# Transposing keys and queries 128 columns at a time, with an earlier place for them in the attention steps

## The reference

```python
block, window = (32, 16)
k_sum = k.reshape(B, H, nb, block, D).max(axis=3)      # 24 blocks of 32 keys
v_sum = v.reshape(B, H, nb, block, D).mean(axis=3)
scores_l = scale * q @ k.T, kept where |i - j| < window
scores_s = scale * q @ k_sum.T + log(block)
a = softmax over both; out = a @ concat(v, v_sum)
```

## Time and profile before

| engine | busy us | share of the span | instructions |
|---|---|---|---|
| PE (matmul) | 550.4 | 89% | 3031 |
| PEld (weight load) | 453.7 | 74% | 3032 |
| DVE | 299.4 | 49% | 726 |
| ACT | 260.9 | 42% | 509 |
| POOL | 106.3 | 17% | 152 |

### The profile page before, as it was taken

The page is one execution under the profiler, slowest core; times in us unless marked ns, Lnnn a source line. Parts: engine busy times, 40 slices in busy tenths (PEclk is TensorE's granted clock), DMA queues, the critical chain, the costliest instruction groups (busy, mean ns, idle before and its releaser), DMA issues.

```text
span 616.8 us, 10082 instructions
## 1 busy us (share of the span) xinstructions
PE 550.4 (89%) x3031; PEld 453.7 (74%) x3032; DVE 299.4 (49%) x726; ACT 260.9 (42%) x509; POOL 106.3 (17%) x152
## 2 busy tenths in 40 slices
PE   2687878796299999999997999999999999999996
PEld 1576667675178888888885888888888888888884
DVE  3645644554675521255126576674355445344441
ACT  2636656544346412144214455543433333433332
POOL 3253562100711200013101522300000000000000
PEclk9969998985599999999999999999999999999999
DMA  8949695202765541134411633300100000100001
GB/s 175 210 90 202 144 290 143 86 2 69 251 219 191 169 175 34 51 115 162 149 53 53 206 102 103 104 18 18 68 0 0 0 0 0 68 0 0 0 0 68
DMA packets 47790, 58.37 MB, mean 95 GB/s; under 512 B 21448, under 2 KB 33736, under 8 KB 47376
## 3 DMA queue, kind: packets, MB, share of 16 engines
q1 hardware_dynamic: 36464, 24.12, 16.7%
q0 software_dynamic: 8640, 29.53, 14.5%
q10 hardware_dynamic: 2656, 4.34, 2.1%
HBM read 41.83 MB, written 14.94 MB: 92 GB/s over the span
## 4 chain that ended last, share of the span: by engine, by line
PE 84%; ACT 5%; DVE 4%; DMA 3%; issue 2%; SPq 0%; POOL 0%; ACTq 0%; DVEq 0%
PE bank L569 76%; ACT SM L1262 2%; PE bank L573 2%; PE bank L634 2%; PE bank L730 2%; DMA TAU<-in_moe_tau 1%; PE bank L708 1%; DMA x_grouped<-XALL,POS 1%; ACT QT L1225 1%; DVE SM L892 1%; DVE VSUM L877 1%; PE bank L799 1%; DMA XG<-x_grouped 1%; ACT XT L1249 1%; ACT KTC L1219 0%
## 5 line engine op out<-in xcount | busy, mean ns | idle before, releaser
L569 PE MATMUL bank<-X2H,WIH 128*128 (+1 forms) x192 | 77.1, 402 | 2.8 <-DVEq L1184 2.8
L569 PE MATMUL bank<-X2H,WIL 128*128 (+1 forms) x192 | 76.6, 399 | 0.0
L569 PE MATMUL bank<-X2L,WIH 128*128 (+1 forms) x192 | 76.5, 398 | 0.0
L569 PE MATMUL bank<-WOH,GH 128*128 128x512 f32 x192 | 75.7, 394 | 0.0
L569 PE MATMUL bank<-WOL,GH 128*128 128x512 f32 x192 | 75.6, 394 | 0.0
L569 PE MATMUL bank<-WOH,GL 128*128 128x512 f32 x192 | 75.6, 394 | 0.0
L573 PE MATMUL bank<-IDENT,KQRAW 128*64 128x128 f32 x192 | 31.6, 311 | 28.7 <-ACT KTC L1219 12.5
L1380 ACT ACTIVATE CC<-CC 128x512 f32<-128x512 f32 x48 | 30.4, 633 | 59.4 <-DVE CC L1173 59.4
L1375 ACT ACTIVATE UU<-bank 128x512 f32<-128x512 f32 x48 | 28.7, 597 | 57.8 <-PE bank L569 57.8
L1171 DVE TENSOR_SCALAR TT<-UU 128x512 f32<-128x512 f32 x48 | 20.4, 426 | 66.6 <-ACT UU L1375 66.6
L1182 DVE TENSOR_TENSOR GL<-GG,GH 128x512 fp32r<-128x512 f32 x48 | 33.2, 692 | 37.1 <-ACT GH L1386 37.1
(11 more groups left out here) (218 smaller groups left out, 1028.2 us busy)
## 6 DMA issues: line engine op xcount, KB each, us to landing
RAW<-in_moe_w POOLq DMA_DIRECT2D x16, 512.0 KB, 6.2
x_grouped<-ZERO POOLq DMA_DIRECT2D x4, 1280.0 KB, 6.3
RAW<-in_moe_w SPq DMA_DIRECT2D x8, 512.0 KB, 7.4
RAW<-in_moe_w_in POOLq DMA_DIRECT2D x16, 256.0 KB, 3.4
RAW<-in_moe_w_out POOLq DMA_DIRECT2D x16, 256.0 KB, 3.3
V<-in_v SPq DMA_DIRECT2D x16, 240.0 KB, 4.9
XG<-x_grouped SPq DMA_DIRECT2D x14, 256.0 KB, 2.7
KQRAW<-in_k SPq DMA_DIRECT2D x16, 192.0 KB, 6.2
```

Source lines behind the costliest of these rows:

```text
L569: return pe.matmul(o, l, r, start=start, stop=stop)
```

## The change

The list of jobs loses `k_both` and `q_both`. `k_0`, `k_1`, `q_0` and `q_1` each transpose one head's 768 positions by three transposes of 128 x 128, whose upper 64 partitions are the even positions and whose lower 64 are the odd ones. ACT copies each in two instructions of 64 x 384. In every step PE runs the jobs first, before `scores(s + 1)`, and ACT ends them before `exps(s + 1)`. `tokens` and `logits` of the first batch get steps of their own from 13 to 23; two `tokens` jobs of the second batch go into step 23. The sums of squares move behind the last job. The tau transfer moves behind the values of pair 0, and DVE's reciprocal of it moves to its use in the expert stage. The keys of pair 0 are spread by DVE for the first four tiles (`k_first`) and by POOL for the other eight. POOL's first fills change order. `first_means` adds halves five times instead of one strided reduction. (The embeddings' job moves from step 2 to 5.)

```diff
-    for kind in ("k_0", "k_1", "k_both", "q_0", "q_1", "q_both"):
+    X_STEPS = (13, 16, 19, 20, 21, 22)
+    for kind in ("k_0", "k_1", "q_0", "q_1"):
         job(-1, kind, 0)
     for step in range(NG_ATT):
         pair, third = divmod(step, CUTS)
+        if third < 2 and pair + 1 < NPAIR:
+            for e in range(2):
+                job(step, ("k_%d", "q_%d")[third] % e, pair + 1)
+        if step == 5:
+            job(step, "emb", 0)
+        for u in range(NT):
+            if step == X_STEPS[u]:
+                job(step, "tokens", u)
+            if step == X_STEPS[u] + 1:
+                job(step, "logits", u)
...
+    for u in (NT, NT + 1):
+        job(NG_ATT - 1, "tokens", u)
     for u in range(NT, NU):
         job(NG_ATT, "logits", u)
+        if u + 2 < NU:
+            job(NG_ATT, "tokens", u + 2)
...
         load_k(0)
-        sp.dma_start(TAU[:, 0:1], ...).then_inc(sem("tau_in"), 16)
         sp.wait_ge(sem("v_ready"), 1)
         load_v(0)
+        sp.dma_start(TAU[:, 0:1], ...).then_inc(sem("tau_in"), 16)
...
         def spread_keys(p):
+            first = PER if p == 0 else 0
+            pool.wait_ge(sem("job_out"), JOB_AT["k_1", p] + 1)
...
+        pool.wait_ge(sem("k_pads"), 1)
+        spread_keys(0)
+        pool.memset(ZERO[:], 0.0).then_inc(sem("zero"), 1)
...
-                for j in range(2):
-                    for k in range(2):
-                        at = (j * 2 + k) * P
-                        m = transposed(ps[0:D, at:at + P], arg, which, e, k, j)
+                for c in range(S // (2 * P)):
+                    m = pe.transpose(ps[:, c * P:(c + 1) * P], KQRAW[:, arg % 3, which, e, c * P:(c + 1) * P], IDENT[:])
...
             if third == 0:
-                pe.wait_ge(sem("k_win"), p + 1)
+                pe.wait_ge(*((sem("k_win"), p + 1) if p else (sem("k_first"), 1)))
+            if s == 1:
+                pe.wait_ge(sem("k_win"), 1)
...
         for s in range(NG_ATT):
+            run_jobs(s)
             if s + 1 < NG_ATT:
                 scores(s + 1)
-            run_jobs(s)
             probs_t(s)
...
-        dve.wait_ge(sem("tau_in"), 16)
         dve.tensor_tensor_reduce(EN[0:NE, :], ...)
-        dve.reciprocal(TAU[:, 1:2], TAU[:, 0:1]).then_inc(sem("dv"), 1)
...
-            link(dve.tensor_reduce(VSUM[rows, :], VRAW[rows, 0, :].rearrange("p (t d) -> p d t", d=D), AX, ALU.add))
+            half = BLOCK * D // 2
+            while half >= D:
+                link(TT_(VRAW[rows, 0, 0:half], VRAW[rows, 0, 0:half], VRAW[rows, 0, half:2 * half], ALU.add))
+                half //= 2
...
+        def keys(ps, p, e):
+            for odd in range(2):
+                i = act.activation(KTC[e * D:(e + 1) * D, p % 2, PAD + odd:PAD + S + odd:2],
+                                   ps[odd * D:(odd + 1) * D, 0:S // 2], ACT.Copy)
+            return i
...
         for s in range(NG_ATT):
+            end_jobs(s)
             if s + 1 < NG_ATT:
                 exps(s + 1)
-            end_jobs(s)
         end_jobs(NG_ATT)
+        for u in range(NU):
+            act.activation(XSQ[:], XALL[:, u, :], ACT.Square, accum_out=XSS[:, u:u + 1]).then_inc(sem("xss"), 1)
+            act.wait_ge(sem("xss"), u + 1)
```

More of the change, by code:

```diff
@@ L281, in build @@
         pair, third = divmod(step, CUTS)
-        if step == 2:
+        if third < 2 and pair + 1 < NPAIR:
+            for e in range(2):
+                job(step, ("k_%d", "q_%d")[third] % e, pair + 1)
+        if step == 5:
             job(step, "emb", 0)
-        done = [2 * (pair - PAIRS) + i for i in range(2)] if PAIRS <= pair < PAIRS + 3 else []
-        late = [2 * (pair - 1 - PAIRS) + 1] if PAIRS < pair < PAIRS + 4 else []
-        if third == 0:
-            for u in late:
+        for u in range(NT):
+            if step == X_STEPS[u]:
+                job(step, "tokens", u)
+            if step == X_STEPS[u] + 1:
                 job(step, "logits", u)
-            if pair + 1 < NPAIR:
-                for kind in ("k_0", "k_1", "k_both"):
-                    job(step, kind, pair + 1)
-        elif third == 1:
-            if pair + 1 < NPAIR:
-                for kind in ("q_0", "q_1", "q_both"):
-                    job(step, kind, pair + 1)
-        else:
-            for u in done:
-                job(step, "tokens", u)
-            for u in done[:1]:
-                job(step, "logits", u)
-    job(NG_ATT, "tokens", NT)
+    for u in (NT, NT + 1):
+        job(NG_ATT - 1, "tokens", u)
     for u in range(NT, NU):
-        if u + 1 < NU:
-            job(NG_ATT, "tokens", u + 1)
         job(NG_ATT, "logits", u)
-    assert len(JOBS) == 1 + 6 * NPAIR + 2 * NU
+        if u + 2 < NU:
+            job(NG_ATT, "tokens", u + 2)
+    assert len(JOBS) == 1 + 4 * NPAIR + 2 * NU
     def jobs_of(step):
@@ L439, in _ @@
         pool.memset(V2[:, :, :, :, D + 1:], 0.0).then_inc(sem("v_ready"), 1)
+        pool.memset(KTC[:, :, 0:PAD], 0.0)
+        pool.memset(KTC[:, :, PAD + S:], 0.0).then_inc(sem("k_pads"), 1)
         scale = 1.0 / math.sqrt(D)
@@ L915, in x_out @@
                 ALU.mult).then_inc(sem("x"), 1)
-        block_max(0)
         first_windows()
@@ L1214, in _, with queries @@
         act.preload_act_table(ACT.Exp)
-        def keys(ps, p, e, c0, n):
-            rows = slice(e * D, (e + 1) * D)
-            return act.activation(KTC[rows, p % 2, PAD + c0:PAD + c0 + n].rearrange("p (c j) -> p j c", j=2),
-                                  ps.rearrange("p (j c) -> p j c", j=2), ACT.Copy)
-        def queries(ps, p, e, t0, n):
-            rows = slice(e * D, (e + 1) * D)
-            return act.activation(QT[rows, p % 2, t0:t0 + n, rows].rearrange("p t (c j) -> p j t c", j=2),
-                                  ps.rearrange("p (j t c) -> p j t c", j=2, t=n), ACT.Copy)
+        def keys(ps, p, e):
[3 more added lines that the diff above has]
+            return i
+        def queries(ps, p, e):
+            rows = slice(e * D, (e + 1) * D)
+            for odd in range(2):
+                i = act.activation(QT[rows, p % 2, :, e * QTILE + odd:(e + 1) * QTILE:2],
+                                   ps[odd * D:(odd + 1) * D, 0:S // 2].rearrange("p (t c) -> p t c", t=TILES), ACT.Copy)
+            return i
         def end_job(n, kind, arg):
```

62 lines of the change are left out of this document (22 added, 40 removed).

## The result

| | before | after |
|---|---|---|
| median of four runs, us | 622.44 | 590.38 |
| lowest and highest run, us | 614.5, 625.0 | 586.06, 591.04 |
| profiled execution, us | 618.4 | 590.14 |
| its span, us | 616.8 | 588.6 |

The changed kernel takes 0.955 of the time of the kernel before (95% interval 0.944 to 0.966). It is faster, and 590.4 us lies inside the range of 584 to 611, 5.6 us under the value of 596. The profiled span is 28.2 us shorter, where the sum had 23.6. (The median before was 620.03 us over three runs; the fourth took 624.86 us, so it is 622.44 here, and the medians differ by 32 us.

The account below looks back on a forecast made before the run. No engine is full; the order of PE's jobs and ACT's copies costs the time. Terms -8.2, -13.9, +1.1, -2.9, -3.7 sum to -27.6; two 2 us allowances give 594.8, plus the median's 1.6: 596 us, range 584 to 611.

Parts of the forecast that it names:

- the sum: Whole kernel, against the profiled 618.4 us: stretches add to -27.6 us, and 23.6 are left after allowances.
- steps 4 to 14: Attention loop: a pair takes 9.0 us, the stretch 32.8 instead of 40.98 us, so -8.2 us.
- steps 14 to 20: Attention steps with tokens and logits: two pairs at 9.7 us and one late even pair, 21.0 from 34.87, -13.9 us.
- `tokens` is a fifth of PE's step (0.44 us): Steps 14 to 20: tokens cost PE 0.44 us, with logits (1.03 us) one step later, in the pair's last step.
- The allowances: Set against the gain: 2 us for half clock in token steps and 2 us for transfers, reckoned at 187 GB/s.
- The start: Up to step 4: ACT copies first keys at 6.9, step 4 begins at 39.9 instead of 43.61; -3.7, between 0 and -7.
- The tail: After the loop: 9.5 instead of 12.45 us, a quarter at half clock, -2.9; moved squares cost nothing, 2.7 us cover left.
- Step 20 to the last `pv`: End of the attention, with logits and tokens in its steps: 15.9 instead of 14.84 us, +1.1 us.
- Transfers: Rival, attention loop: transfers set the pace at 10.2 us per pair over five pairs, 602 us; chance 0.20.
- Waits come back: Rival, 11 job steps: late keys and ACT's copies cost 1 us each, no start gain; 610, 605 to 612; chance 0.14.
- Half clock through the attention: Rival, PE in the loop: the clock falls to 1.2 GHz, PE binds at 15.4 us per pair, 636 us; chance 0.06.
- The drain after a table load: Rival, ACT's chain after the logits: two table switches end 2.8 us later against 2.7 of cover, about 597 us; chance 0.02.

Follow-up runs that it names:

- experiment 1: Changed kernel with PE's jobs behind the next scores and ACT's copies behind the exponentials again, both orders undone: 603.56 us, ratio 0.972 to the kernel before.
- experiment 3: Changed kernel with only PE's order undone, jobs behind the next scores, ACT still ending them before its exponentials: 587.83 us, ratio 0.951 to the kernel before.
- experiment 4: Kernel of Experiment 5 with ACT's order undone, exponentials first and then the jobs' copies: 628.43 us, ratio 1.017 to the kernel before.
- Experiment 5: Changed kernel with the tokens job (third job) of steps 13, 16 and 19 behind the next scores on PE: 588.23 us, ratio 0.949 to the kernel before.
- experiment 10: Changed kernel with tau fetched ahead of pair 0's values again and DVE waiting for it before the embeddings' norms: 593.77 us, ratio 0.961 to the kernel before.
- experiment 11: Changed kernel with each tile's squares back beside its tokens copy in the attention steps: 592.74 us, ratio 0.958 to the kernel before.
- experiment 12: Changed kernel with the squares computed twice behind the last job, 24 instead of 12: 597.41 us, ratio 0.966 to the kernel before.
- experiment 2: Changed kernel with the cut undone, six jobs per pair of four 64-column transposes, in the new order: 594.61 us, ratio 0.959 to the kernel before.

## Why the prediction was right, and where it was off

**The mechanism.** PE did stand for copies that ACT had queued behind exponentials, and the changed order takes that away. Pair 3 takes 8.99 us (9.0 forecast), POOL's even pair 10.5 (10.6). But I had put the gain down to two things at once, the jobs ahead of the scores on PE and half the transposes. Experiments 1, 3 and 4 show that of the two orders ACT's is the one that gains: undoing PE's costs nothing, undoing both costs 7 to 15 us, and undoing ACT's alone makes the kernel slower than the kernel before. The order is not the whole gain, though. With both orders undone the kernel is still some 17 us under the kernel before, and those have been taken apart only in part: undoing the cut in the new order costs about 4 us, and undoing the early tau about 3. The old cut with the old orders, ACT's new order alone in the kernel before, and the tokens' old steps (in the stretch with the largest gain, 12.3 us) weren't run, so how these 17 us divide isn't shown. Nor do the parts add up, because each exposes or hides another wait.

**The term that was off most: steps 4 to 14, -6.1 instead of -8.2, and steps 14 to 20, -12.3 instead of -13.9.** The step that failed is "`tokens` is a fifth of PE's step (0.44 us)". The tokens are the third job of steps 13, 16 and 19, with two banks. They wait 1.45 to 1.48 us for ACT's copy of the queries, which itself stands behind the exponentials of the last scores, and the next scores are queued behind them. That is the wait of the earlier trace rows, kept in three steps; I had written that nothing in a step waits for ACT's copies, which holds for two jobs only. The sum for steps 4 to 14 left the tokens of step 13 out altogether. Up to the first scores of pair 4 that stretch went as forecast (4.1, 9.0 and 10.5 us for 4.2, 9.0 and 10.6); from there to those of pair 5 it took 12.64 us instead of 9.0. The tokens and their wait are 2.1 us of the excess: from the first transposes of step 13 to its scores are 69.53 - 66.72 = 2.81 us, and 0.71 in a step with two jobs. The other part is half clock, which lasted until about 64.3, behind the 2.81 us in which PE waited for POOL; by the row under *The allowances* I estimate 1.2 to 1.8 us for it (1.2 by the next pair, which takes 11.45 us at full clock, and 1.8 by the mean clock, 0.14 x 12.64). In steps 14 to 20 the sum was 1.5 us short. Experiment 5 takes most of the tokens' wait away, and its three pairs give back 1.5, 0.6 and 0.7 us.

**The start: -6.9 instead of -3.7.** ACT copied the first keys at 6.9 and the first scores came at 11.2, as forecast. The keys of pair 1 did not come where they were forecast: I had them at 16.3 and let the move of tau shift them by half a microsecond at most, but SP issued them 2.1 us earlier than before (9.42 for 11.49), and PE had them at 14.5. So the means started at 18.6 and not at 20.5; the first product with values came at 29.2 for 30.0. The larger part of the miss lies behind it: from that product to step 4 are 7.5 us, where I had 9.9 and the kernel before took 11.55 (7.8, 7.1 and 7.6 us in the three other traces with this start). PE was at half clock through 28.8 to 42.5 while working before, and after only until 34.2. I priced durations in this stretch as they stood. What shortens the half-clock stretch wasn't tried by itself. Step 4 begins at 36.4 to 38.8 in the four traces with this start, so the miss of 3.2 us is 1.1 to 3.5. The tau move is worth 1.3 to 3.6 us at the first product, by experiment 10.

**The tail.** Step 20 to the last `pv` cost nothing instead of 1.1. Behind it the gain was 1.6 instead of 2.9: half clock came from 112.1 on, in the course of these six logits and four tokens, and the mean is 0.64, where I had taken a quarter at half clock. The squares took 9.0 us as forecast, with 2.28 us of cover left (2.7 forecast); experiments 11 and 12 show both sides of it, no cost in either place and 7 us past the cover. The 1.5 us from the last logits to the first expert product were not in the sum and weren't traced to a part; it isn't the squares' place, since 1.1 of them stay when that is undone (19.7 us, experiment 11).

**The allowances.** I took 4 us for clock and transfers. The clock over 36.70 to 94.11 is 0.97, and over 71.57 to 94.11 it is 1.00, so the clock took 1.2 to 1.8 us (that one pair) of its 2. The transfers don't pace the loop: a stretch of 12.6 us moved 279 GB/s, where the allowance reckoned with 187.

```profile
60.29:72.93 12.64, 10.88 (x108) 9.62 (x109) 6.79 (x35) 8.64 (x22) 3.46 (x6) 0.86 1.11 279
```

**The rivals.** *Transfers* fell by that row, and by no wait for keys in pairs 5 to 7. *Waits come back* was right in kind (tokens, `k_win`) and small in size. *Half clock through the attention* didn't come, but other orders of the same computation had more of it: a mean of 0.88 over the first 150 us in experiment 4, and 0.79 over the attention in the longest execution of experiment 1. So it was a real neighbour. (Its own terms give 635 us, and not 636.) *The drain after a table load* fell: the root starts 129.98 - 128.69 = 1.29 us after its load began, the weights' copy 131.50 - 130.21 = 1.29 us after the second. The Trainium skill (ScalarE: Activation LUTs, section What ACT_TABLE_LOAD costs) adds about 1380 ns to each; in experiment 12, where ACT's time is exposed, the two loads still start 1.53 us apart with a root between them, and nothing of that size is seen.

## What to carry to other kernels

When two engines hand work to each other through a few buffers, look first at what the copying engine has queued ahead of the copy; here that one order was worth more than the order of the engine that waits, and with it in place the cut was worth no more than about 4 us. Then undo the parts in pairs too, since one part can stand in for another: with both orders undone, more than half of the gain was still there. Count the jobs of every step against the buffers, and not only those of the typical step: three steps out of twenty-four kept such a wait. Trace the same code more than once before you explain a microsecond or two: four traces of one start differ by 2.5 us. And price a stretch at the clock it will have, since a shorter wait ahead of it also moves where the half clock ends.

## What the runs showed of the hardware that wasn't expected

- Transposes of 64-column and 128-column blocks run at the same pace (four in 0.63 us, eight in 1.06 us of experiment 2; six of 128 columns in 0.87), so half as many transposes cost half.
- PE can be busy 10.60 of 10.81 us on logits of 8 columns and transposes and still be at half clock in a good part of it (mean 0.64 from 108.96 to 119.77). It was busy without a break from 108.96 until the clock fell at 112.1, so being busy did not keep the clock here.
- One order of the same instructions had a mean clock of 0.91 over the attention and another 0.88 (experiment 4), or 0.79 in the longest execution of experiment 1.
- Before its first change of clock a trace can give 1.00 while PE runs at half pace: transposes follow each other by 0.24 us up to 19 us, and by 0.11 in the loop.
- The issue of the 128-partition tau transfer behind the values takes 3.13 us on SP (6.25 to 9.38), and the keys of pair 1 are issued behind it. The same issue took 1.27, 3.00 and 4.51 us in the three other traces with this start.
